# New step lists for four engines in a fused attention, MLP and expert kernel

## The reference

```
# 1: gated linear attention, for every t of a sequence, 8 heads of 48 channels
a_n = a * min(|a|, 0.999) / (|a| + 1e-6)          # complex gate a = a_re + i a_im
S = a_n[t] * S + k[t] v[t]^T                       # S complex, k and v real
y[t] = q[t] . Re(S)
# 2: MLP of 2048
h = x @ w_in;  g = max(h, 0) + alpha * min(h, 0);  x2 = g @ w_out
# 3: top-1 experts, 8 of them, 1024 wide, for tokens with x2 @ w_skip > 0
e = argmax(x2 @ w_gate);  gate_w = softmax(x2 @ w_gate)[e]
out = x2 + gate_w * (max(x2 @ w1[e], 0) @ w2[e])   # other tokens: out = x2
```

## Time and profile before

| | us |
|---|---|
| median of 3 runs (955.61 to 956.36) | 955.71 |
| the profiled execution's own time | 956.43 |
| its span | 954.7 |
| PE busy | 747.9 (78%) |
| DVE busy | 699.5 (73%) |
| ACT busy | 368.3 (39%) |
| POOL busy | 51.7 (5%) |
| mean granted clock of PE | 0.921 |

### The profile page before, as it was taken

How to read it: one execution, slowest core, us unless ns; L and a number is a source line. 1 busy time by engine, 2 the same in 40 slices (tenths; PEclk the granted TensorE clock), 3 DMA queues, 4 the chain that set the end, 5 groups by cost and what they waited for, 6 DMA issues and landing times. The chain is left out here.

```text
span 954.7 us, 16060 instructions
## 1 busy us (share of the span) xinstructions
PE 747.9 (78%) x5478; PEld 721.5 (76%) x5478; DVE 699.5 (73%) x1230; ACT 368.3 (39%) x804; POOL 51.7 (5%) x48
## 2 busy tenths in 40 slices
PE   1342356987888998788798978979999825989897
PEld 1342356987887898788798978879999825989896
DVE  6967988988999899899979989985433272543433
ACT  5452233444434543533453453344443221422231
POOL 1000000000000000000000000000000002332322
PEclk9999667999999899999989999999999955989999
DMA  6552343253323424334242442324220098354300
GB/s 190 175 159 74 97 122 89 58 139 99 99 72 90 141 65 126 115 81 110 62 139 67 116 125 71 81 56 138 75 73 1 19 346 294 119 207 145 103 30 18
DMA packets 82431, 104.71 MB, mean 110 GB/s; under 512 B 15990, under 2 KB 68384, under 8 KB 82336
## 3 DMA queue, kind: packets, MB, share of 16 engines
q1 hardware_dynamic: 80544, 99.69, 35.4%
q0 software_dynamic: 1792, 3.76, 1.2%
HBM read 61.04 MB, written 12.19 MB: 77 GB/s over the span
## 5 line engine op out<-in xcount | busy, mean ns | idle before, releaser
L524 PE MATMUL out_ps<-w_out_hi,g_parts 128*128 128x394 f32 x768 | 225.2, 350 | 26.2 <-DVE g_parts L933 26.2
L514 PE MATMUL mlp_ps<-xT,w_in_hi 128*128 128x384 f32 x768 | 207.9, 352 | 19.0 <-DMA xT<-y_parts 8.6
L524 PEld LDWEIGHTS out_ps<-w_out_hi,g_parts 128*128 128x128 f32 x768 | 145.7, 193 | 30.1 <-DVE g_parts L933 30.0
L514 PEld LDWEIGHTS mlp_ps<-xT,w_in_hi 128*128 128x128 f32 x768 | 141.7, 195 | 25.3 <-issue 12.8
L928 DVE SCALAR_TENSOR_TENSOR g<-mlp_ps,slope_side,bent 128x384 f32<-128x384 f32 x128 | 78.6, 615 | 84.8 <-ACT bent L666 76.7
L524 PE MATMUL out_ps<-w_out_lo,g_parts 128*128 128x394 f32 x384 | 133.6, 348 | 0.0
L666 ACT ACTIVATE bent<-mlp_ps,bend_size 128x384 f32<-128x384 f32 x128 | 73.9, 577 | 150.9 <-PE mlp_ps L514 150.5
L514 PE MATMUL mlp_ps<-xT,w_in_lo 128*128 128x384 f32 x384 | 131.7, 343 | 0.0
L1308 PE MATMUL mlp_ps<-xT_e,w_sb 128*128 128x128 f32 x624 | 78.0, 288 | 8.6 <-issue 7.9
L1308 PEld LDWEIGHTS mlp_ps<-xT_e,w_sb 128*128 128x128 f32 x624 | 76.8, 204 | 10.4 <-issue 10.4
L672 ACT ACTIVATE g_parts<-g 128x384 fp32r<-128x384 f32 x128 | 66.3, 518 | 35.3 <-DVE g L928 35.3
(11 more groups left out here) (147 smaller groups left out, 1076.1 us busy)
## 6 DMA issues: line engine op xcount, KB each, us to landing
kq<-qk_dec SPq DMA_DIRECT2D x96, 144.0 KB, 3.0
w_sb<-in_w SPq DMA_DIRECT2D x8, 1536.0 KB, 7.6
w_raw<-in_w SPq DMA_DIRECT2D x8, 1536.0 KB, 11.8
gates<-in_a SPq DMA_DIRECT2D x24, 384.0 KB, 4.1
qk_raw<-in_qk SPq DMA_DIRECT2D x24, 384.0 KB, 4.4
xT<-y_parts SPq DMA_DIRECT2D x48, 144.0 KB, 2.8
v_nat<-in_v SPq DMA_DIRECT2D x24, 192.0 KB, 4.3
out<-x SPq DMA_DIRECT2D x8, 576.0 KB, 3.1
```

What stands on the lines that cost most here:

```text
L514: last = pe.matmul(ps[:, 0:HT], w_in_v[s][:, kk, f * P:(f + 1) * P], xT[n.p][:, kk, m, :], start=(kk == 0 and j == 0), stop=(kk == KT - 1 ...
L524: last = pe.matmul(out_ps[i][:, 0:DL], g_parts[:, f % 4, s, i * P:(i + 1) * P], w_out_v[m][:, f, :], start=(f == 0 and j == 0), stop=(f == ...
```

## The change

All that follows is one edit.

- The four `step` lists are laid anew. `decay_qk`, `scale_gates`, `within`, `across`, `carry_products`, `values`, `back_k`, `mask_scores` and `scale_state` are cut into parts that the lists place apart, and a wait for an earlier DVE result stands now ahead of the instruction that reads it, not behind the one that wrote it.
- `move_qk` moves the real and the imaginary half apart, five DMAs each, the first when the first half of `qk_dec` is made. `move_state` goes ahead of `move_y`.
- In the preload the splitting of the weights is mixed into the gate products in other portions.
- `gates` and `qk_raw` lie in two buffers (`arena`) that outlive phase 1; in pass 7, once the last q and k are decayed, SP loads w1 and w2 of expert 0 into them. `x2`, `x_in`, `x_kept_rows` and `y` share one buffer, `rows`.
- SP no longer waits for the last store at the end of phase 1; POOL does ahead of the first gather. SP loads expert 3 when the first gather has landed.
- Routing: two scans in place of the doublings, fewer casts, conversions on POOL, the table from fp32r operands (132 columns wide, in 24 matmuls) in place of fp32 ones (66 columns).

```diff
             def move_qk(h, c, r):
-                sp.wait_ge(qk_made, made)
-                for r in range(2):
-                    for p0, n, t0, nt, row, slot in OP_MOVES:
+                sp.wait_ge(qk_made, made)          # made = 2 * chunk + r + 1
+                for p0, n, t0, nt, row, slot in OP_MOVES:
...
+            def fetch_first_expert():
+                sp.wait_ge(qk_made, 2 * NC * HALVES)
+                sp.dma_start(arena[0][:, :].rearrange("p (k f) -> p k f", k=KT),
+                             w1[0:1].rearrange("e (k p) f -> p (e k) f", p=P)).then_inc(first_loaded[0], 16)
+                sp.dma_start(arena[1][:, :].rearrange("p (f d) -> p f d", f=NFE),
+                             w2[0:1].rearrange("e (f p) d -> p (e f) d", p=P)).then_inc(first_loaded[1], 16)
+            step(Half(0, HALVES - 1), True, False, fetch_first_expert)
             store_x2(Half(0, HALVES - 1))
-            sp.wait_ge(x2_stored, val(32 * HALVES + 1))
...
             def multiply(h, done, x, y_re, y_im, prod_a, prod_b):
+                if done == 0:
+                    dve.wait_ge(a_normed, val(chunk_no(h, NC)))
+                else:
+                    dve.wait_ge(prod_step, val(h.n * PROD_STEPS + done))
                 dve.tensor_tensor(prod_a, x, y_re, ALU.mult).then_inc(prod_step, 1)
                 dve.tensor_tensor(prod_b, x, y_im, ALU.mult).then_inc(prod_step, 1)
-                dve.wait_ge(prod_step, val(base + 2))
+            def combine(h, done, new_re, new_im, prod_a, prod_b):
+                dve.wait_ge(prod_step, val(h.n * PROD_STEPS + done + 2))
                 dve.tensor_tensor(new_re, prod_a[:, 0], prod_b[:, 1], ALU.subtract).then_inc(prod_step, 1)
                 dve.tensor_tensor(new_im, prod_a[:, 1], prod_b[:, 0], ALU.add).then_inc(prod_step, 1)
-                dve.wait_ge(prod_step, val(base + 4))
...
-            sp.wait_ge(table_full, 1)
+            sp.wait_ge(x_gathered, 16)
             load_w1(BODY - 1)
...
+            dve.tensor_tensor_scan(sums[:, :], flat(goes_on), mlp_ps[1][:, 0:NT * EXPERTS], 0.0,
+                                   ALU.mult, ALU.add).then_inc(step, 1)
```

More of the change, by code:

```diff
@@ L452, in ended, with scores, turn_k, is_carried @@
                 return ins.then_inc(att_full[att(h, name, c)[0]], 1)
[L454 to L470, removed]
+            def scores(h, c, half):
+                ps = begin(h, f"s{half}", c)
+                for n in range(PAIRS):
+                    slot = PAIRS * half + n
+                    last = pe.matmul(ps[:, n * CH:(n + 1) * CH], kq[:, slot, 1, :], kq[:, slot, 0, :],
+                                     start=True, stop=True)
+                ended(last, h, f"s{half}", c)
+            def turn_k(h, c, half):
+                if half == 0:
+                    pe.wait_ge(qk_moved, val((chunk_no(h, c) + 1) * (32 * len(OP_MOVES))))
+                ps = begin(h, f"k{half}", c)
+                for n in range(PAIRS):
+                    last = pe.transpose(ps[:, n * ROWS:(n + 1) * ROWS], kq[:, PAIRS * half + n, 1, :],
+                                        ident[0:ROWS, 0:ROWS])
+                ended(last, h, f"k{half}", c)
+            def is_carried(h, c):
+                return not (h.p == 0 and c == 0)
+            def y_of(ps, hd):
+                at = UP * (hd % 2)
+                return ps[at:at + D, hd // 2 * CH:(hd // 2 + 1) * CH]
             def values(h, c):
@@ L546, in step @@
[L546 to L550, removed]
-                values(h, 1)
[L552 to L558, removed]
-                values(h, 2)
-                for f in range(13, NF + LAG):
-                    of_mlp(f)
+                n, nxt = h.plus(-1), h.plus(1)
@@ new lines, in step @@
+                decay(h, 2, 0)
+                if more:
+                    multiply_within(nxt, 2)
+                mask_scores(h, 1, 0)
+                if more:
+                    combine_within(nxt, 2)
+                mask_scores(h, 1, 1)
+                if more:
+                    multiply_within(nxt, 3)
+                if mlp_too:
+                    low_g(n, 5)
+                if more:
+                    combine_within(nxt, 3)
+                if mlp_too:
+                    join_g(n, 7)
@@ new lines, in step @@
+                if more:
+                    multiply_within(nxt, 4)
+                decay(h, 2, 1)
+                if more:
+                    combine_within(nxt, 4)
+                if mlp_too:
+                    low_g(n, 6)
+                if more:
+                    multiply_within(nxt, 5)
+                if mlp_too:
+                    join_g(n, 8)
+                if more:
+                    combine_within(nxt, 5)
+                if mlp_too:
+                    join_g(n, 9)
@@ L1004, in step @@
+                if mlp_too:
+                    low_g(n, 12)
+                if more:
+                    carry(nxt, 4)
+                    carry(nxt, 5)
                 low_y(h, 2)
                 add_state(h, 2)
[L1006 to L1011 removed]
+                if mlp_too:
+                    join_g(n, 14)
                 if more:
```

827 lines of the change are left out of this document (511 added, 316 removed).

## The result

| | before | after |
|---|---|---|
| median of 4 runs each | 956.04 (955.61 to 958.53) | 889.92 (884.72 to 892.74) |
| the profiled execution's own time | 956.43 | 892.74 |
| its span | 954.7 | 891.0 |
| DVE busy | 699.5 | 673.1 |
| PE busy, mean granted clock | 747.9, 0.921 | 731.8, 0.945 |

The changed kernel takes 0.9297 of the time of before, 95% interval 0.9251 to 0.9343. From profile to profile it is 63.7 us less; 79.7 were forecast. 889.9 lies within the range, but outside the 866 to 886 of the likeliest case.

A forecast was written before the change was run, and what follows sets the result against it. DVE was taken to bound the loop of six passes, over half the time. Savings in eight terms summed to -79.7 us from 956.43, giving 876 us; likeliest case 866 to 886 (0.56), range 861 to 904.

The forecast's parts named there:

- The six passes: Main loop: 82.0 us a pass falls to 73.5, saving 51.0 us; bounds 72 and 78 us a pass.
- the list of margins: Loop: due times of other engines' work against DVE's list, half a dozen margins under 1 us; 1.5 us of waits allowed.
- The prediction's own sign of being wrong: Loop: wrong if DVE waits over 2 us a pass for q and k, moves or states, or separated dependents cost as before.
- Rival 1: Loop: margins missed, late moves and states cost 4 us more a pass; 900 us, chance 0.20.
- DVE's floor: Loop: DVE's busy time without tails behind about 26 dependent neighbours, 74.5 - 2.3 = 72.2 us a pass.
- Rival 2: Seven passes: an instruction put between two dependents saves nothing, 33 us lost; 909 us, chance 0.08.
- Pass 0: First pass: 70.5 us before, laid out at 62.7, taken as 64, minus 6.5 us (4 to 9).
- Pass 7, last MLP and the barrier: End of phase 1: pass 7 minus 1.5 us, last MLP unchanged, SP's wait for the store's landing minus 3.8.
- Routing: Between the phases: scans, fewer steps and the fp32r table make routing 6.9 us shorter.
- Gather: First gather, 8.94 us before, takes 3.0 without weight loads beside it, minus 6.0 us.
- Slots: Phase 2: loads of expert 3 and w2 of expert 4 cross the second gather, plus 2.5 us (0 to 5).
- Rival 4: Loop: SP's order ties chunk 1's moves to chunk 0's k v product; slower, 988 us at 15.5 a chunk, chance 0.04.

The follow-up runs named there:

- qk_early: Changed kernel with SP asking for q and k of chunk 1 of the next half ahead of the state moves and the x2 store; 875.59 us, ratio 0.9149.
- qk_rotated: qk_early with PE's loop turned so that its jump back stands ahead of `down(13)`; 866.36 us, ratio 0.9069 to the kernel before.
- sp_waits: Changed kernel with SP's wait for the last x2 store put back at the end of phase 1; 894.33 us, ratio 0.9336.
- qk_split: qk_early with DVE's split of expert 0's w2 moved behind its copy of the first gathered rows; 873.51 us, ratio 0.9129.
- store_behind: Changed kernel with the load of q, k and v of chunk 1 right ahead of the x2 store, not behind it; 878.71 us, ratio 0.9179.

## Why the prediction was right in kind and 16 us short

- **The six passes**: minus 35.5 us, not 51.0. This is nearly the whole miss of 16.0 us. The other terms were off by up to 2.6 us each and cancel to 0.5, which is luck. The step that failed is the list of margins. "q and k of chunk 1 are asked for at 3.3, behind the store of x2, and are due at 7.6" named the place, and gave the load 4.3 us; it was asked for at 4.2 and took 5.9, since the 1.2 MB of the store were ahead of it. The 4.4 us of the loads in the kernel before could have told that 4.3 leave no slack. And "PE's longest stop is 1.7 us ahead of `up(2)`, so I expect no fall of the clock" had neither the 2.8 us stop behind the late k nor the 3.1 us jump of the loop, of which the trace of the kernel before showed 1.4 and 1.7 us; the granted clock was 0.95 to 0.98 in five of the six passes. The prediction's own sign of being wrong came true: DVE waited for q and k for more than 2 us in passes 2, 4 and 6. With the first repaired the passes took 73.5 us in the mean (qk_early), with both the 72 of the forecast's lower bound (qk_rotated).
- **Rival 1** (4 us a pass) was therefore half right: SP's order cost 2.5 us a pass (14.9 us over the six, by qk_early), at one place. Its sentence "after a late one, what follows has slack" was wrong for `bent` and for PE.
- **DVE's floor**: 72.2 us forecast, 71.4 measured. The difference of the earlier trace rows held at all 11 places of a pass: 0.37 against 0.48 to 0.49 us behind the seven longest products, and 0.11 to 0.12 us apart behind the four shorter ones. The prediction set this against "The DRAIN you can't avoid" on the page "VectorE: DVE Perf Modes" of the Trainium skill. That section also says that a next instruction which is not held starts earlier; the trace agrees with this sentence (0.37 us). It does not agree with the section's finding that a semaphore behind each instruction costs nothing extra: here the reader that waits for the one ahead starts 0.12 us later. Rival 2 had priced all 26 neighbours at 33 us. With 11 of them put back the loop lost under 1 us in the profiles and the kernel 3 to 5 in the medians, so the 33 look too many, but no run put all of them back.
- **Preload**: minus 5.0 us, 6.5 forecast. **Pass 0**: minus 8.4, not 6.5: the 62.7 laid out was nearer than the 64 taken.
- **Pass 7, last MLP and the barrier**: from 642.1 to 766.75 before, from 593.0 to 713.57 after, minus 4.1; 5.3 forecast. sp_waits prices the barrier at 4.0 (3.8 forecast), and the traces at 3.7 (4.19 us from the end of SP's last issue to the start of routing before, 0.45 after), so pass 7 gave 0.4 us at most, not 1.5.
- **Routing** up to the gather's start on GpSimd: 27.7 us before, 20.65 after, minus 7.05; 6.9 forecast. A scan of 192 elements takes 0.55 us (0.6 taken), an fp32r matmul of 132 columns 0.25 us at a granted clock of 0.50 (0.23 taken).
- **Gather**: minus 3.6 us, not 6.0. "Nearest row is the scatter, 2.6 us" was the mis-sized term: the scatter never meets a split, the first gather does. So it was in the kernel before too: 8 of its 14 gathers, the first among them, start inside a split and take 3.3 us on GpSimd, the other 6 take 1.0. Without loads beside it it took 5.34 us, of which some 2.2 are the split's, as qk_split shows.
- **Slots**: nothing lost where 2.5 us were forecast. From the gather's landing to the end of the span it is 151.3 us before and 151.4 after.
- **Rival 4** (the tie through SP's order) did not show: PE waits for the moves of q and k 1.1 us at most in a pass of the loop.

The Trainium skill's page "SBUF — State Buffer", section "Who interferes with whom", says that a DVE instruction with two SBUF inputs and a GpSimd instruction that reads SBUF exclude each other for the whole instruction. The trace agrees, if the gather is taken as an instruction that reads SBUF, where its indices lie: its 3.27 us on GpSimd end 1.1 us behind the split, about its length alone (1.0). The same section infers that such a two-input instruction does not hold up the making of a DMA's descriptors. Whether the gather was held up in that or in reading its indices, no run here tells.

## What to carry to other kernels

A due time in a list laid out by hand must count the bytes that its queue has ahead of it, not the issue time alone: a load that is wanted soon goes ahead of a store that nobody waits for. Look where a loop's jump falls on an engine that has little slack, and turn the loop until it falls where the engine waits anyway. A saving in an engine's list need not show in the time: 1.1 us put back between the products of a pass lengthened passes 2, 4 and 6 by 0.3 to 0.5, since waits behind them shrank. And look in the trace of the kernel before for the price of every load and every gap at the place itself, not at the nearest kin: the 4.4 us of the loads, the gap at the jump and the gathers of 3.3 us all stood there.

## Unexpected on this hardware

- PE's jump back cost 3.1 us behind the last matmul, with no engine waited for; ahead of a wait of 1.6 us it cost nothing that shows.
- With the same loop written out, one gap of PE far behind it, in the slots, was 8.8 us long (3.6 to 5.2 in the other runs); the cause is open.
- An indirect DMA took GpSimd 1.0 us, or 3.3 when DVE was in a two-input instruction of 3.35 us.
- Asking for q and k, 0.4 MB, some 1.2 us sooner, ahead of a store of 1.2 MB and not behind it, was worth over 11 us of 890 (store_behind).
